# Key transposes moved ahead of the tail's scores in slot 0, with another order of loads, weight splits and the last stores, in a fused attention and two-layer gated network

## The chip, the cores and the metric

One core of a Trainium2 chip runs the whole program. The metric is the device time of one execution in microseconds (us). The engines that matter are TensorE (PE in the rows), VectorE (DVE), ScalarE (ACT), GpSimd (POOL) and SyncE (SP), which issues nearly all DMAs; ACT issues a few weight loads. A matmul streams one operand through weights loaded before and writes PSUM. Each engine runs its own instruction list in order, and semaphores tie the lists together.

## The reference

```python
def _attn_ref(q, k, v):                      # (8, 8, 576, 64) each
    k_p = k.reshape(B, H, Sp, pool, D).mean(axis=3)     # pool 8: 72 keys
    v_p = v.reshape(B, H, Sp, pool, D).mean(axis=3)
    scores = scale * np.matmul(q, k_p.transpose(0, 1, 3, 2))
    scores = scores - np.max(scores, axis=-1, keepdims=True)
    attn = np.exp(scores)
    attn = attn / (np.sum(attn, axis=-1, keepdims=True) + 1e-09)
    return np.matmul(attn, v_p)
...
x = attn_out.transpose(0, 2, 1, 3).reshape(B * S, H * D)    # 4608 x 512
h = x @ w_in1                                # 512 -> 2048
g = where(h >= 1, h, where(h <= -1, 0, (h + 1) ** 2 / 4))
x = g @ w_out1                               # 2048 -> 512
h = x @ w_in2;  g = h / (1 + exp(-h));  out = g @ w_out2
```

## The kernel before

All products of the two layers are made in three passes over operands split into a high and a low part: `hi*hi`, `hi*lo`, `lo*hi` (`three_passes`, L676 to L678). ScalarE makes the high part (`split_high`, `split_input`, `gate_high`), VectorE or GpSimd subtracts it from the raw value for the low part (`split_low`, `gate_low`).

The 4608 tokens form nine blocks of 512; there are 18 block passes, nine for layer 1 and nine for layer 2. A block pass has 16 steps `s`. In each, PE makes hidden chunk `s` (12 matmuls into `ps_h`) and the output product of chunk `s-2` (12 matmuls into the four banks of `ps_y`), while DVE, ACT and POOL turn `ps_h` into the gate's high and low parts. The layers hand over through `y_dram`, the attention hands over through `x_dram`.

The attention of batch `b` is spread over the layer 1 pass of block `b`. Its work is cut into pieces, and the table `PIECES` gives each piece a slot; there are two slots for each step. Each batch has five units `u`: unit 0 is the tail of 64 tokens of this batch, units 1 to 4 are pairs of heads of the next batch. "S" is a unit's scores (PE), maximum and subtraction (`take`, DVE), exponential (ACT), and in the slot behind, `normalise` and `turn_probs` (DVE). "V" is its product with the values (PE) and `copy_output` (ACT), "Q" turns the next queries (`turn_queries`, DVE), and "K" transposes the next batch's pooled keys on PE (`turn_keys`, L604) and copies them to `kT` (`copy_keys`, ACT). S of unit `u` sits in slot `5u`, V in `5u+7`; K sits in slot 2. All share the two PSUM banks `ps_a`; scores use columns 0 to 287 of each, and the keys have been turned into columns 0 to 287 of bank 1, which is why `turn_keys` waits until the tail's scores are taken out. Probabilities go out to `p_dram` and come back transposed as `pT` (`put_probs`, `take_probs`), since the DMA does part of the turning.

Block 0 has an order of its own (`first_block`, `first_gates`, the `FIRST_*` tables): weights are still being loaded and split, and four attention units are made before it. In it, PE walks the slots through `first_slot`, and ACT and DVE follow in `first_gates` and then in `one_block(..., start=6)`. `FIRST_LOW_DVE` says after which step DVE splits which weight piece.

SP's list sets the order of the DMAs: `first_attention_dmas` and `attention_dmas` for the two kinds of block, then `store_y`. SP waits in place, so a DMA behind a waiting one is issued later. The second layer's weights are loaded during block 8 through a ring of three places (`load_weight`), 24 pieces (`SWAP_TAIL`) in that block; then SP loads the first input of layer 2 (`load_x(blocks, y_dram, 0, half)`). A block's result leaves `ps_y` through two buffers of `y_sb`, ACT's and DVE's in turn (`copy_y`, L924 and L1154); each second copy waits until the store out of its buffer has landed.

Of the kernel before, what the change touches and what calls it, by code (L numbers as in the profile page):

```python
# [8 lines left out]
ACT = mybir.ActivationFunctionType  # L9
AXIS_X = mybir.AxisListType.X  # L10

P = 128
BLOCK = 512
POOL = 8
PAIRS = 4
# [13 lines left out]
UNITS = 5  # L29
PIECES = {2: [("K", 0), ("Q", 0)]}  # L30
# [36 lines left out]
FIRST_LOW_DVE = {4: (10,), 5: (14, 16), 7: (19,), 8: (21,), 9: (23,), 10: (25,), 11: (27,), 12: (29,),  # L67
# [12 lines left out]
def build(nc, q, k, v, w_in1, w_out1, w_in2, w_out2, x_dram, y_dram, out):  # L80
# [12 lines left out]
    with ExitStack() as ctx:  # L93
# [73 lines left out]
        early_o = [ps_h[:, 0, :], ps_h[:, 1, :], ps_h[:, 0, :], ps_y[:, 0, :]]  # L167

# [70 lines left out]
        def unit(b, u):  # L239

            return 5 * b + (PAIRS + 1 + u)
# [120 lines left out]
        def _(sp):  # L362
# [115 lines left out]
            def first_attention_dmas():  # L478
# [18 lines left out]
                put_probs(0, 3)  # L497
                sp.wait_ge(kv_added, 12)
                load_kv(k, 2, 0)
                store_pair(0, 1, 1)  # L500
                take_probs(0, 3)
# [11 lines left out]
                sp.wait_ge(kv_added, 18)  # L513
                load_kv(v, 2, 0)
# [47 lines left out]
            store_y(0, 0, 0)  # L562
            with sp.Fori(1, batches - 1) as b:
                attention_dmas(b, (b + 2) % batches)
                store_y(b, b, 0)
# [7 lines left out]
            for i in range(SWAP_TAIL):  # L573
                load_weight(sp, W_PIECES + i)
            for half in range(2):
                load_x(blocks, y_dram, 0, half)
            store_y(blocks - 1, blocks - 1, 0)
# [13 lines left out]
            store_y(2 * blocks - 1, blocks - 1, 1)  # L591
# [8 lines left out]
        def _(pe):  # L600
# [232 lines left out]
        def _(act):  # L833
# [20 lines left out]
            def copy_keys(b, u):  # L854
                act.wait_ge(kT_made, b + (PAIRS + 1))
                for r in range(2):
                    rows = slice(r * dim, (r + 1) * dim)
                    turned = ps_a[rows, 1, 0:PAIRS * keys].rearrange("p (c k) -> p c k", k=keys)
                    nc.scalar.activation(kT[rows, :, r, :], turned, ACT.Copy).then_inc(kT_copied, 1)
# [25 lines left out]
            task_of = {"K": copy_keys, "S": exponential, "V": copy_output}  # L885

            def attention_slot(b, slot, most):
                for kind, u in PIECES.get(slot, ()):
                    if kind in task_of and u < most and not (kind == "K" and most == 1):
                        task_of[kind](b, u)  # L890

# [41 lines left out]
            def first_gates():  # L933
# [11 lines left out]
                attention_slot(0, 2, UNITS)  # L945
# [8 lines left out]
            def one_block(B, layer, units=0, loads=lambda s: (), more=True, start=0):  # L954
                for s in range(start, FC):
                    before, behind = slots_of(B, s)
                    gate_begin(B, s, layer)
                    for slot in before:
                        attention_slot(B, slot, units)
# [11 lines left out]
                copy_y(B)  # L971
# [68 lines left out]
        def _(dve):  # L1040
# [104 lines left out]
            def copy_y(B, units):  # L1145
                if units > 0:
                    dve.wait_ge(x_stored, 80 * B + 16 * units)
                for i in range(2):
                    if i == 0:
                        dve.wait_ge(y_done, B * 3 + 2)  # L1150
                    else:
                        dve.wait_ge(l2_done, B * FC + FC)
                    dve.wait_ge(y_stored[1], B * 32 + 16 * (i + 1))
                    nc.vector.tensor_copy(y_sb[:, 1, :], ps_y[:, 2 * i + 1, :]  # L1154
                                          ).then_inc(y_copied_dve, 1)
# [23 lines left out]
            def one_block(B, layer, units=0, loads=lambda s: (), more=True, start=0):  # L1179
# [15 lines left out]
                copy_y(B, units)  # L1195
# [140 lines left out]
```

## Time and profile before

| what | value |
|---|---|
| three runs | 1694.07, 1694.46, 1699.36 us; median 1694.46 |
| the profiled execution | 1694.82 us, its span 1693.0 us |
| PE busy | 1673.6 us, 99% of the span |
| DVE, ACT, POOL busy | 685.2, 507.5, 545.3 us |
| TensorE's granted clock, mean | 0.998 |
| from the tail's scores of block 2 to those of block 3 | 98.54 us |

The span runs from the first to the last instruction; the remaining 1.8 us of the execution lie outside it. PE being busy at 99% says that only its few idle stretches, its time at a lower clock, and the time before its first and behind its last matmul can be shortened without taking matmuls away.

### The profile page before, as it was taken

How to read it: one execution, taken by the hardware profiler on the slowest of the kernel's cores; microseconds unless marked ns; L12 is line 12 of the kernel's file. 1: busy time of each engine (PE TensorE's matmuls, PEld its weight loads, DVE VectorE, ACT ScalarE, POOL GpSimd, SP SyncE). 2: the span in 40 equal slices, each digit the busy share in tenths (PEclk: the TensorE clock that was granted, in tenths of full speed). 3: DMA queues.
4: the chain of work that ended last, by engine and by line, in shares of the span. 5: the costliest groups of instructions: out<-in, count | busy, mean ns of one | idle time of the engine just before them, and what ended most of it. 6: DMA issues, size and time to landing. Idle time of an engine off the chain costs nothing.

```text
span 1693.0 us, 21063 instructions
## 1 busy us (share of the span) xinstructions
PE 1673.6 (99%) x7588; PEld 1355.9 (80%) x7588; DVE 685.2 (40%) x900; ACT 507.5 (30%) x856; POOL 545.3 (32%) x418
## 2 busy tenths in 40 slices
PE   8999999999999999999999999999999999999998
PEld 6777777787877778788887888888888888888887
DVE  7866656475765647442464221212121212121211
ACT  5442232332323233232344222322232223222222
POOL 6653524244352434322222222222222222222221
PEclk9999999999999999999999999999999999999999
DMA  8654525344352534420123110101010101010000
GB/s 217 165 152 97 127 69 121 95 100 110 82 129 65 121 96 100 110 62 1 59 97 112 32 50 1 50 0 50 0 50 0 50 0 50 0 50 0 25 0 25
DMA packets 139799, 114.99 MB, mean 68 GB/s; under 512 B 86676, under 2 KB 95892, under 8 KB 139764
## 3 DMA queue, kind: packets, MB, share of 16 engines
q1 hardware_dynamic: 138036, 111.38, 24.6%
q10 hardware_dynamic: 1728, 3.15, 0.6%
q8 instruction: 21, 0.34, 0.1%
q14 instruction: 14, 0.11, 0.0%
HBM read 74.65 MB, written 39.85 MB: 68 GB/s over the span
## 4 chain that ended last, share of the span: by engine, by line
PE 93%; DVE 2%; DMA 2%; SPq 1%; issue 0%; ACT 0%; POOL 0%; DVEq 0%; ACTq 0%
PE ps_h L676 15%; PE ps_y L676 15%; PE ps_h L677 15%; PE ps_h L678 15%; PE ps_y L678 15%; PE ps_y L677 15%; PE ps_a L646 2%; PE ps_a L617 2%; DMA second_k<-in_k_dram 1%; PE ps_a L633 0%; DMA pT<-p_dram 0%; DVE win_lo L1047 0%; SPq L397 0%; SPq L378 0%; DMA x_raw<-y_dram 0%
## 5 line engine op out<-in xcount | busy, mean ns | idle before, releaser
L1269 POOL TENSOR_TENSOR g_lo<-g_tmp,g_hi 128x512 fp32r<-128x512 f32 x286 | 369.9, 1293 | 1100.2 <-ACT g_hi L915 1100.2
L676 PE MATMUL ps_h<-x_hi,win_hi 128*128 128x512 f32 x1144 | 451.5, 395 | 0.5 <-DVE g_tmp L1139 0.3
L677 PE MATMUL ps_h<-x_lo,win_hi 128*128 128x512 f32 x1144 | 446.2, 390 | 0.0
L678 PE MATMUL ps_h<-x_hi,win_lo 128*128 128x512 f32 x1144 | 445.9, 390 | 0.0
L1143 DVE TENSOR_TENSOR g_tmp<-g_tmp,ps_h 128x512 f32<-128x512 f32 x144 | 99.0, 688 | 577.4 <-ACT g_tmp L905 577.4
L676 PEld LDWEIGHTS ps_h<-x_hi,win_hi 128*128 128x128 f32 x1144 | 215.2, 188 | 58.1 <-issue 12.2
L678 PEld LDWEIGHTS ps_h<-x_hi,win_lo 128*128 128x128 f32 x1144 | 215.2, 188 | 45.4
L677 PEld LDWEIGHTS ps_h<-x_lo,win_hi 128*128 128x128 f32 x1144 | 215.1, 188 | 43.0
L915 ACT ACTIVATE g_hi<-g_tmp 128x512 fp32r<-128x512 f32 x286 | 180.5, 631 | 225.7 <-DVE g_tmp L1139 121.4
L676 PE MATMUL ps_y<-g_hi,wout_hi 128*128 128x512 f32 x576 | 227.8, 395 | 1.0 <-POOL g_lo L1269 1.0
L678 PE MATMUL ps_y<-g_hi,wout_lo 128*128 128x512 f32 x576 | 224.3, 389 | 0.0
L677 PE MATMUL ps_y<-g_lo,wout_hi 128*128 128x512 f32 x576 | 224.3, 389 | 0.0
L676 PE MATMUL ps_y<-wout_hi,g_hi 128*128 128x512 f32 x576 | 224.1, 389 | 0.0
L677 PE MATMUL ps_y<-wout_lo,g_hi 128*128 128x512 f32 x576 | 224.1, 389 | 0.0
L678 PE MATMUL ps_y<-wout_hi,g_lo 128*128 128x512 f32 x576 | 224.1, 389 | 0.0
L905 ACT ACTIVATE g_tmp<-ps_h 128x512 f32<-128x512 f32 x144 | 86.1, 598 | 420.5 <-PE ps_h L678 420.5
L908 ACT ACTIVATE g_tmp<-g_tmp 128x512 f32<-128x512 f32 x142 | 89.7, 632 | 363.3 <-DVE g_tmp L1132 363.3
L1132 DVE TENSOR_SCALAR g_tmp<-ps_h 128x512 f32<-128x512 f32 x142 | 96.9, 683 | 207.8 <-PE ps_h L678 207.5
L676 PEld LDWEIGHTS ps_y<-g_hi,wout_hi 128*128 128x128 f32 x576 | 108.1, 188 | 35.8 <-issue 13.0
L678 PEld LDWEIGHTS ps_y<-g_hi,wout_lo 128*128 128x128 f32 x576 | 108.1, 188 | 23.1
L677 PEld LDWEIGHTS ps_y<-wout_lo,g_hi 128*128 128x128 f32 x576 | 108.3, 188 | 22.5
L676 PEld LDWEIGHTS ps_y<-wout_hi,g_hi 128*128 128x128 f32 x576 | 108.1, 188 | 22.4
(121 smaller groups left out, 1246.1 us busy)
## 6 DMA issues: line engine op xcount, KB each, us to landing
p_dram<-x_raw SPq DMA_DIRECT2D x28, 384.0 KB, 2.3
y_dram<-y_sb SPq DMA_DIRECT2D x36, 256.0 KB, 2.1
x_raw<-y_dram SPq DMA_DIRECT2D x18, 512.0 KB, 4.2
out_dram<-y_sb SPq DMA_DIRECT2D x36, 256.0 KB, 2.1
kv_raw<-in_k_dram SPq DMA_DIRECT2D x15, 576.0 KB
kv_raw<-in_v_dram SPq DMA_DIRECT2D x15, 576.0 KB
x_raw<-x_dram SPq DMA_DIRECT2D x16, 512.0 KB, 4.1
q_pair<-in_q_dram SPq DMA_DIRECT2D x120, 64.0 KB, 4.8
```

The costliest lines, as they stand in the source:

```text
L617: last = mm(banks[:, t // 2, at:at + 2 * keys], qT[:, t * P:(t + 1) * P], kT[:, c, :, :].rearrange("p r k -> p (r k)"), start=True, stop=True)
L646: last = mm(bank[r * dim:(r + 1) * dim, :], v_sum[:, 2 * c + r, :], probs[:, r], start=True, stop=True)
L676: mm(dst, w_h, a_h, start=first, stop=False)
L677: mm(dst, w_h, a_l, start=False, stop=False)
L678: return mm(dst, w_l, a_h, start=False, stop=last)
L905: nc.scalar.activation(t, ps_h[:, s % 2, :], ACT.Sigmoid).then_inc(sigmoid_done, 1)
L908: nc.scalar.activation(t, t, ACT.Square, bias=1.0).then_inc(square_done, 1)
L915: nc.scalar.activation(g_hi[:, s % G_BUFS, :], t, ACT.Copy).then_inc(g_hi_done, 1)
L1132: nc.vector.tensor_scalar(t, bank_of(B, s), -1.0, 1.0, ALU.max, ALU.min).then_inc(ramp_done, 1)
L1143: nc.vector.tensor_tensor(t, t, h, ALU.mult).then_inc(g_done, 1)
L1269: nc.gpsimd.tensor_tensor(g_lo[:, s % G_BUFS, :], gate_place(B, s), g_hi[:, s % G_BUFS, :].bitcast(F32), ALU.subtract).then_inc(g_lo_done, 1)
```

## The change

The order is changed in six places.

1. `PIECES`: K goes from slot 2 to slot 0, ahead of the tail's scores. The keys are turned into columns 288 to 431 of both `ps_a` banks, two head pairs in each, so PE no longer waits there for the scores to be taken. ACT copies them in slot 1.
2. In block 0, SP issues the store of pair 1 and the three loads of `pT` for unit 3 ahead of a load of pooled keys' input that waits for POOL.
3. Behind block 0, SP issues the four `y` stores ahead of the load of values that waits for POOL's last sum.
4. In block 0, DVE splits weight piece 16 one step later, and ACT runs the slots in front of a step's gate ahead of `gate_begin` (not behind it).
5. In block 8, SP loads the first input of layer 2 ahead of the last six of the 24 weight pieces.
6. The last block's result is copied into the four chunks of `x_raw`, not the two buffers of `y_sb`, so that no copy waits for a store.

```diff
-PIECES = {2: [("K", 0), ("Q", 0)]}
+PIECES = {0: [("K", 0)], 2: [("Q", 0)]}
...
-FIRST_LOW_DVE = {4: (10,), 5: (14, 16), 7: (19,), 8: (21,), 9: (23,), 10: (25,), 11: (27,), 12: (29,),
+FIRST_LOW_DVE = {4: (10,), 5: (14,), 6: (16,), 7: (19,), 8: (21,), 9: (23,), 10: (25,), 11: (27,), 12: (29,),
...
+        turned_keys = ps_a[:, :, 4 * keys:6 * keys].rearrange("p g (c k) -> p g c k", k=keys)
...
                 put_probs(0, 3)
+                store_pair(0, 1, 1)
+                take_probs(0, 3)
                 sp.wait_ge(kv_added, 12)
                 load_kv(k, 2, 0)
-                store_pair(0, 1, 1)
-                take_probs(0, 3)
...
-                sp.wait_ge(kv_added, 18)
-                load_kv(v, 2, 0)
+
+            def store_last_y():
+                for d in range(4):
+                    sp.wait_ge((y_copied_act, y_copied_dve)[d % 2], 2 * (2 * blocks - 1) + d // 2 + 1)
+                    at = (blocks - 1) * BLOCK + d * P
+                    sp.dma_start(out[at:at + P, :], x_raw[:, d, :]).then_inc(y_stored[d % 2], 16)
...
             store_y(0, 0, 0)
+            sp.wait_ge(kv_added, 18)
+            load_kv(v, 2, 0)
...
-            for i in range(SWAP_TAIL):
+            for i in range(SWAP_TAIL - 6):
                 load_weight(sp, W_PIECES + i)
             for half in range(2):
                 load_x(blocks, y_dram, 0, half)
+            for i in range(SWAP_TAIL - 6, SWAP_TAIL):
+                load_weight(sp, W_PIECES + i)
...
             def turn_keys(b, u):
                 pe.wait_ge(kv_added, 12 * b + 6)
-                pe.wait_ge(scores_taken, unit(b, 0))
+                pe.wait_ge(o_copied, 5 * b)
                 for c in range(PAIRS):
-                    last = transpose_keys(ps_a[:, 1, c * keys:(c + 1) * keys], c)
+                    last = transpose_keys(turned_keys[:, c // 2, c % 2, :], c)
...
             def copy_keys(b, u):
                 act.wait_ge(kT_made, b + (PAIRS + 1))
+                act.wait_ge(scores_taken, unit(b, 0))
...
+                if ("K", 0) in PIECES.get(slot - 1, ()) and most > 1:
+                    copy_keys(b, 0)
...
-            def copy_y(B):
+            def copy_y(B, more):
...
-                    act.wait_ge(y_stored[0], B * 32 + 16 * (i + 1))
-                    nc.scalar.activation(y_sb[:, 0, :], ps_y[:, 2 * i, :], ACT.Copy
-                                         ).then_inc(y_copied_act, 1)
+                    if more:
+                        act.wait_ge(y_stored[0], B * 32 + 16 * (i + 1))
+                    elif i == 0:
+                        act.wait_ge(x_lo_done, 2 * blocks * KC)
+                    dst = y_sb[:, 0, :] if more else x_raw[:, 2 * i, :]
+                    nc.scalar.activation(dst, ps_y[:, 2 * i, :], ACT.Copy).then_inc(y_copied_act, 1)
...
                     before, behind = slots_of(B, s)
+                    if start:
+                        for slot in before:
+                            attention_slot(B, slot, units)
                     gate_begin(B, s, layer)
-                    for slot in before:
-                        attention_slot(B, slot, units)
+                    if not start:
+                        for slot in before:
+                            attention_slot(B, slot, units)
```

VectorE's `copy_y` is changed as ScalarE's is.

Order on PE at the start of a pass of the batch loop, before. L633 is the tail's scores, L604 the key transposes, and the two are one hidden chunk apart:

```order
L622 ISA
L633 MATMUL ps_a<-kT,qT 64x144 x4
L676 MATMUL ps_h<-x_hi,win_hi 128x512
L677 MATMUL ps_h<-x_lo,win_hi 128x512
...
L608 ISA
L609 REGISTER_ALU
L604 MATMUL ps_a<-ident,k_sum 128x72 x4
L691 ISA
L676 MATMUL ps_h<-x_hi,win_hi 128x512
```

The same place now (L615 are the transposes, L644 the scores):

```order
L619 ISA
L620 REGISTER_ALU
L615 MATMUL ps_a<-ident,k_sum 128x72 x4
L633 REGISTER_ALU
L644 MATMUL ps_a<-kT,qT 64x144 x4
L687 MATMUL ps_h<-x_hi,win_hi 128x512
```

The transposes have moved one hidden chunk forward, in front of the scores, and no wait for the scores stands between chunks 1 and 2 any more.

Order on SP at the end of block 0 before. The names are the DRAM and SBUF tensors; the `kv_raw` rows are loads of keys or values, the `y_sb` row the block's four stores:

```order
L371 DMA kv_raw<-in_k_dram 72x4x512
L420 DMA x_dram<-y_sb 128x512
L437 DMA x_raw<-x_dram 128x2x512
L371 DMA kv_raw<-in_v_dram 72x4x512
L524 DMA y_dram<-y_sb 128x512 x4
```

And now:

```order
L374 DMA kv_raw<-in_k_dram 72x4x512
L423 DMA x_dram<-y_sb 128x512
L440 DMA x_raw<-x_dram 128x2x512
L531 DMA y_dram<-y_sb 128x512 x4
L374 DMA kv_raw<-in_v_dram 72x4x512
```

The load of values, with its wait for POOL, has gone behind the stores. Order on DVE in steps 5 and 6 of block 0, before (L1047 are weight splits, L1132 begins a gate, L1090 turns queries):

```order
L1058 TENSOR_TENSOR prob<-ps_a,row_max 128x8x72
L1047 TENSOR_TENSOR win_lo<-w_early,win_hi 128x512
L1047 TENSOR_TENSOR win_lo<-w_raw,win_hi 128x512
L1063 TENSOR_REDUCE row_sum<-prob 128x8
...
L1132 TENSOR_SCALAR g_tmp<-ps_h 128x512
L1090 STREAM_TRANSPOSE qT<-q_pair 128x512
```

And now:

```order
L1072 TENSOR_TENSOR win_lo<-w_early,win_hi 128x512
L1088 TENSOR_REDUCE row_sum<-prob 128x8
...
L1157 TENSOR_SCALAR g_tmp<-ps_h 128x512
L1115 STREAM_TRANSPOSE qT<-q_pair 128x512
...
L1083 TENSOR_TENSOR prob<-ps_a,row_max 128x8x72
L1072 TENSOR_TENSOR win_lo<-w_raw,win_hi 128x512
```

The second split (piece 16) has moved behind the next unit's subtraction.

## Rows read from the trace of the kernel before

**Rows 1.** Page, part 1: busy time, share, instructions of each engine.
```profile
PE 1673.6 (99%) x7588; PEld 1355.9 (80%) x7588; DVE 685.2 (40%) x900; ACT 507.5 (30%) x856; POOL 545.3 (32%) x418
```
**Rows 2.** Waits of PE: us in total, times, longest (four of the 14 rows).
```profile
PE ps_a L604 <- DVE prob L1058: 2.2, 1, 2.2
PE ps_a L617 <- ACT y_sb L878: 2.0, 1, 2.0
...
PE ps_a L646 <- DMA pT<-p_dram: 1.1, 1, 1.1
PE ps_y L676 <- POOL g_lo L1269: 1.0, 1, 1.0
```
**Rows 3.** Chain of work, the tail's scores in blocks 1, 2, 3: start, us, what.
```profile
133.68 1.12 PE ps_a L633 x8
...
236.53 1.12 PE ps_a L633 x8
...
335.07 1.12 PE ps_a L633 x8
```
**Rows 4.** Windows: length, busy (x) by engine, PEclk, DMA share, GB/s.
```profile
140.00:145.00 5.00, 4.88 (x17) 3.82 (x18) 4.71 (x7) 1.12 (x2) 1.27 (x1) 0.66 0.00 0
```
**Rows 5.** Timeline, 130 to 140 us (block 1 begins): start, us, what, [idle before <-releaser].
```profile
130.14 0.32 SPq L371 DMA_DIRECT2D kv_raw<-in_v_dram  x1
...
130.50 7.68 SPq L524 DMA_DIRECT2D y_dram<-y_sb  x4
...
137.13 0.69 DVE L1154 COPY y_sb<-ps_y 128x512 f32<-128x512 f32 x1 [6.75 <-DMA y_dram<-y_sb]
...
137.74 0.68 DVE L1132 TENSOR_SCALAR g_tmp<-ps_h 128x512 f32<-128x512 f32 x1
...
139.92 0.47 PE L604 MATMUL ps_a<-ident,k_sum 72*128 72x72 f32 x4 [2.17 <-DVE prob L1058]
```
**Rows 6.** Timeline, 232 to 241 us, the same place in block 2.
```profile
232.57 4.14 SPq L524 DMA_DIRECT2D y_dram<-y_sb  x4
...
239.15 0.67 DVE L1139 SCALAR_TENSOR_TENSOR g_tmp<-g_tmp,ps_h 128x512 f32<-128x512 f32 x1
...
240.44 0.41 PE L604 MATMUL ps_a<-ident,k_sum 72*128 72x72 f32 x4
...
240.66 0.48 PE L676 MATMUL ps_h<-x_hi,win_hi 128*128 128x512 f32 x1
...
240.98 0.40 PE L677 MATMUL ps_h<-x_lo,win_hi 128*128 128x512 f32 x1
```
**Rows 7.** Timeline, 57 to 84 us, block 0 from step 5 on.
```profile
57.88 4.27 DVE L1047 TENSOR_TENSOR win_lo<-w_raw,win_hi 128x512 fp32r<-128x512 f32 x1
...
60.31 1.28 POOL L1269 TENSOR_TENSOR g_lo<-g_tmp,g_hi 128x512 fp32r<-128x512 f32 x1
...
65.29 0.65 DVE L1132 TENSOR_SCALAR g_tmp<-ps_h 128x512 f32<-128x512 f32 x1
...
83.02 0.70 DVE L1047 TENSOR_TENSOR wout_lo<-w_early,wout_hi 128x512 fp32r<-128x512 f32 x1
```
**Rows 8.** Timeline of SP, 94 to 97 us (block 0).
```profile
94.44 0.31 SPq L371 DMA_DIRECT2D kv_raw<-in_k_dram  x1
...
95.23 1.91 SPq L414 DMA_DIRECT2D pT<-p_dram  x3
```
**Rows 9.** Windows of 100 us: around the change of layer, and inside layer 2.
```profile
814.00:914.00 100.00, 98.92 (x435) 81.08 (x434) 51.41 (x66) 40.79 (x69) 23.23 (x18) 1.00 0.31 102
1078.00:1178.00 100.00, 100.00 (x442) 82.83 (x442) 18.84 (x27) 27.13 (x45) 24.51 (x19) 1.00 0.12 42
```
**Rows 10.** Timeline around 898 us and at the end.
```profile
898.18 1.16 ACT L896 ACTIVATE x_hi<-x_raw 128x512 fp32r<-128x512 f32 x2 [1.96 <-DMA x_raw<-y_dram]
...
1687.80 0.39 PE L678 MATMUL ps_y<-wout_hi,g_lo 128*128 128x512 f32 x1
...
1689.75 0.69 DVE L1154 COPY y_sb<-ps_y 128x512 f32<-128x512 f32 x1 [2.20 <-DMA out_dram<-y_sb]
```

More of the change, by code:

```diff
@@ L590, in _ @@
                 block_dmas(b)
-            store_y(2 * blocks - 1, blocks - 1, 1)
+            store_last_y()
             sp.wait_ge(kv_landed, 16 * (4 * batches - 2))
@@ L855, in copy_keys @@
                 act.wait_ge(kT_made, b + (PAIRS + 1))
+                act.wait_ge(scores_taken, unit(b, 0))
                 for r in range(2):
                     rows = slice(r * dim, (r + 1) * dim)
-                    turned = ps_a[rows, 1, 0:PAIRS * keys].rearrange("p (c k) -> p c k", k=keys)
-                    nc.scalar.activation(kT[rows, :, r, :], turned, ACT.Copy).then_inc(kT_copied, 1)
+                    nc.scalar.activation(kT[rows, :, r, :].rearrange("p (g c) k -> p g c k", g=2),
+                                         turned_keys[rows], ACT.Copy).then_inc(kT_copied, 1)
             def exp_rows(held):
@@ L883, in copy_output @@
                 nc.scalar.activation(dst, src, ACT.Copy).then_inc(o_copied, 1)
-            task_of = {"K": copy_keys, "S": exponential, "V": copy_output}
+            task_of = {"S": exponential, "V": copy_output}
             def attention_slot(b, slot, most):
                 for kind, u in PIECES.get(slot, ()):
-                    if kind in task_of and u < most and not (kind == "K" and most == 1):
+                    if kind in task_of and u < most:
                         task_of[kind](b, u)
+                if ("K", 0) in PIECES.get(slot - 1, ()) and most > 1:
+                    copy_keys(b, 0)
             def split_input(B, half):
@@ L944, in first_gates @@
                 gate_begin(0, 4, 0)
-                attention_slot(0, 2, UNITS)
+                attention_slot(0, 1, UNITS)
                 gate_high(0, 3)
@@ L970, in one_block @@
                         split_high(n)
-                copy_y(B)
+                copy_y(B, more)
             def first_keys(c):
@@ L1143, in gate_end, with copy_y @@
                     nc.vector.tensor_tensor(t, t, h, ALU.mult).then_inc(g_done, 1)
-            def copy_y(B, units):
+            def copy_y(B, units, more):
                 if units > 0:
@@ L1152, in copy_y @@
                         dve.wait_ge(l2_done, B * FC + FC)
-                    dve.wait_ge(y_stored[1], B * 32 + 16 * (i + 1))
-                    nc.vector.tensor_copy(y_sb[:, 1, :], ps_y[:, 2 * i + 1, :]
-                                          ).then_inc(y_copied_dve, 1)
+                    if more:
+                        dve.wait_ge(y_stored[1], B * 32 + 16 * (i + 1))
+                    dst = y_sb[:, 1, :] if more else x_raw[:, 2 * i + 1, :]
+                    nc.vector.tensor_copy(dst, ps_y[:, 2 * i + 1, :]).then_inc(y_copied_dve, 1)
             def first_gates():
@@ L1194, in one_block @@
                     split_input(B + 1)
-                copy_y(B, units)
+                copy_y(B, units, more)
             nc.vector.memset(kT[:], 0.0).then_inc(kT_zero, 1)
```

## Prediction

> **What bounds the kernel now.** The page's busy times come first: PE is busy 1673.6 of 1693.0 us [rows 1], no matmul is taken away, so the change can win only PE's idle time, time at a lower clock, and the tail behind its last matmul. The list of PE's waits, read next, says where the idle time is: four single waits of 2.2, 2.0, 1.1 and 1.0 us, each happening once in the program [rows 2]. None falls in the batch loop from its second pass on. The chain of waits then gives the price of the first one. The tail's scores stand at the same place in each pass, so their distance is the length of a pass: 335.07 - 236.53 = 98.54 us from block 2 to 3, but 236.53 - 133.68 = 102.85 us from block 1 to 2 [rows 3]. Block 1 costs 4.31 us more than its like, though its wait is only 2.2 us. The rest is the clock: between 140 and 145 us the granted clock is 0.66 of full, a mean over stretches at 2.4 GHz and at 1.2 GHz, and 17 matmuls run where 5.00 / 0.2262 = 22 would fit (0.2262 us is 100 us / 442) [rows 4, 9]. It fell right after the 2.17 us of idle.
>
> **The change part by part**, against the profiled execution of 1694.82 us (span 1693.0 and 1.8 around it).
>
> Boundary of blocks 0 and 1 (parts 1 and 3 of the change). PE waits at the key transposes for VectorE's subtraction of the tail's scores. VectorE is late because its gate starts at 137.74, behind the second copy of `y` at 137.13, which sat idle 6.75 us for a store out of its buffer. That store was issued behind a load of values, which SP had held back to 130.14 for POOL's last sum; the four stores took SP 7.68 us from first to last [rows 5]. In block 2, where no such load is ahead, SP needs 4.14 us, and no wait arises [rows 6]. With the stores first, block 1 becomes like block 2. Moving the transposes would remove the named wait alone, but not the late gate, on which hidden chunk 2 waits as well; the two edits have one answer. I take the whole 4.3 us. The bounds: 0 if the stores stay late, 4.31 at most. What is hidden: the values' load now starts some 3 us later, when the last copy is out, and POOL needs it two steps into block 1, which at 98.54 / 16 = 6.2 us a step is over 10 us on; without that cover its lateness would reach PE through POOL's list.
>
> Step 6 of block 0 (part 4). PE waits 2.0 us for ACT's copy of the tail's output [rows 2]. ACT made it behind its gate step, which waited for VectorE's gate begin at 65.29; in front of that VectorE spent 4.27 us on the split of piece 16 [rows 7]. Now the copy goes ahead of the gate step and the split behind the next unit. PE also needs the queries turned by VectorE right behind the gate begin, so the order of ACT alone would give back only part; the split's 4.27 us are the larger term, and 65.29 - 4.27 = 61.0 brings the gate begin forward by more than the wait. I take 2.0. Lower bound 0 (below).
>
> Unit 3's probabilities in block 0 (part 2). PE waits 1.1 us for `pT` [rows 2]. Its loads are issued at 95.23, behind the load of keys' input at 94.44, which itself waited for POOL [rows 8]. Ahead of it, they wait only for the copy of unit 2's output, and do not share the DMA engines with that load. I take the 1.1 and 0.1 for the slower first matmul after a stop: 1.2, between 0 and 1.2. The keys' load slips by about what the store and three loads take to issue, 0.4 + 1.9 us, into POOL's slack.
>
> Change of layer (part 5). ScalarE gets `x_raw` at 898.18 after waiting 1.96 us for a load [rows 10]; the gate's high part of chunk 15 is queued behind it, POOL waits for that, and PE for POOL, 1.0 us [rows 2]. Both following gates are late too. 100 us around this place hold 435 matmuls, 100 us of layer 2 hold 442 [rows 9]: 7 x 0.2262 = 1.6 us. With six weight pieces fewer in front, the load is issued about three steps of 24 matmuls, some 16 us, earlier. I take 1.6 (0 to 1.6). The last six pieces have these 16 us less only by the load's own time; each has a step of slack, so nothing is charged.
>
> The end (part 6). The last matmul starts at 1687.80 and takes 0.39; the last copy starts at 1689.75, having waited 2.20 us for a store [rows 10]. With a place of its own it starts at about 1688.25, and everything behind it is as before: 1.5 us. If four stores so close disturb each other, less: 0.5 as the lower bound.
>
> The loop (part 1). In each of seven blocks the transposes, 240.44 to 240.66, join the scores. The first matmul after them is followed by the next after 0.32 us and not 0.2262 [rows 6]; one such change of kind falls away: 0.09 x 7 = 0.65. Between transposes and scores a new one may arise, so 0 to 1.3, or a loss up to 0.65. The transposes' 0.22 us now stand in front of the scores, and the tail's take, and with it the end of gate 0, come 0.22 to 0.31 us later: 239.15 + 0.67 becomes about 240.1, while chunk 2, which waits for it, starts at about 240.6. The slack of 0.84 shrinks to about 0.5 and holds. ACT's key copies move into a stretch in which it waits for the next gate.
>
> Sum: 4.3 + 2.0 + 1.2 + 1.6 + 1.5 + 0.65 = 11.25 us; 1694.82 - 11.25 = 1683.6 for the profiled execution. The median of the runs is 0.36 below that execution, so 1683.2 us.
>
> The split of piece 16 took 4.27 us while POOL worked without a pause (its row at 60.31 is one of four), and a split of the same size at 83.02 took 0.70 [rows 7]. By the Trainium skill, SBUF — State Buffer, section "SBUF: two separate sides", a VectorE operation with two SBUF inputs and a GpSimd operation that reads SBUF exclude each other for a whole instruction; the trace agrees. By that rule the split can be as long at its new place, since POOL has splits of its own there; the sum would lose up to all of part 4.
>
> **The rivals.**
> A. The split is as long at its new place and delays gate 7 and unit 2's probabilities by 2 to 4.3 us; or the earlier pace of block 0 meets a load that comes no earlier. For it: 4.27 us in a row that has 0.70 elsewhere. Against: the new place has no PE wait near it, and gate 7 is not needed for two steps. Loses 2 to 4.3: 1685.2 to 1687.5, say 1686.2.
> B. The boundary stall stays: the stores land late for another reason, or the gate starts late all the same. For it: four stores are waited for one by one. Against: block 2 does the same in 4.14 us. 1683.2 + 4.3 = 1687.5.
> C. The change of layer gives nothing: the load of 1 MB in front of piece 18 starves ScalarE's next weight split. Against: the ring has a step of slack. 1683.2 + 1.6 = 1684.8, or 1686 with a stall of its own.
> D. Slower: gate 0 falls behind chunk 2 in the batch loop. The slack of 0.84 us is used up by the transposes in front of the scores (a register wait and a new change of kind between them), PE stops by x in each of six passes, and each stop brings the clock down as in block 1, where 4.31 - 2.17 = 2.1 us came on top of the idle time. It costs 6 (x + 2.1) and decides from x = 0.7, where it is 16.8 and outweighs 11.25 by 5.1. With x = 1.0: 1683.8 + 18.6 = 1702.4. Against: 0.31 is the most I find, and it needs over 1.5.
>
> **How the numbers follow.** Forecast 0.72, A 0.13, B 0.05, C 0.04, D 0.06. A measurement of this kernel tells 0.3%, 5.1 us, from no change. The forecast, A, B and C are all more than 5.1 below 1694.5: faster 0.94. D is split between small x (within 0.3%) and larger: same 0.03, slower 0.03. The range takes the forecast with its terms' bounds (1681.5 if the loop gives 1.3 and block 0 another 1 us), A and B: 1681.5 to 1688.0.
>
> **What would show it.** Block 1 as long as block 2, and a granted clock of 1.00 from 140 to 145 us; `y_dram` stores of block 0 over in about 4 us; the PE waits on `pT`, on the tail's copy, on `g_lo` at the change of layer and on VectorE's subtraction gone from the list; 441 or 442 matmuls in the 100 us around the change of layer; the last copy starting 0.1 us behind the last matmul, and the span ending some 3.3 us behind it; block 2 to 3 at about 98.4 us. Wrong: block 2 to 3 above 98.54 (the loop pays), a new PE wait of over 1 us in block 0 (A), or a stretch below full clock.

## The result and the profile after

| | before | after |
|---|---|---|
| runs | 1694.46, 1699.36, 1694.07, 1696.63 us | 1684.07, 1685.51, 1683.99, 1685.45 us |
| median | 1695.55 us | 1684.76 us |
| profiled execution, its span | 1694.82, 1693.0 us | 1684.07, 1682.3 us |

The ratio is 0.9933, with a 95% interval of 0.9914 to 0.9951, so the kernel is faster by more than 0.3%. The profiled executions are 10.75 us apart where the sum gave 11.25. As before [rows 1], the page's part 1 shows no matmul gone. PE is busy 3.1 us less with as many:

```profile
PE 1670.5 (99%) x7588; PEld 1355.7 (81%) x7588; DVE 691.9 (41%) x900; ACT 508.0 (30%) x856; POOL 546.0 (32%) x418
```

The list of PE's waits (us in total, times, longest) answers to [rows 2]. None of the four rows there has a counterpart. The first two rows below are in the opening, and their like was in the list before. The one on `L687` is new and lies behind the change of layer:

```profile
PE ps_a L651 <- DVE prob L1097: 2.8, 1, 2.8
PE ps_h L808 <- POOL ident L1318: 1.5, 1, 1.5
...
PE ps_h L687 <- DVE g_tmp L1168: 0.2, 1, 0.2
```

The chain of work gives the length of a pass as in [rows 3]. From the tail's scores of block 1 to those of block 2 it is now 98.53 us, not 102.85, and from block 2 to 3 98.54, as before:

```profile
130.22 1.12 PE ps_a L644 x8
...
228.75 1.12 PE ps_a L644 x8
...
327.29 1.12 PE ps_a L644 x8
```

The windows of [rows 4] and [rows 9], the columns being busy time (count) of PE, weight loads, DVE, ACT and POOL, then granted clock, DMA share and GB/s. The clock at the boundary is 1.00 where it was 0.66, and 441 matmuls, not 435, run around the change of layer:

```profile
140.00:145.00 5.00, 5.00 (x26) 4.25 (x25) 4.01 (x7) 3.03 (x5) 3.76 (x3) 1.00 0.28 56
814.00:914.00 100.00, 99.80 (x441) 82.32 (x440) 53.59 (x67) 42.44 (x72) 25.49 (x20) 1.00 0.28 94
```

The timeline around 130 us answers to [rows 5]. The four stores are issued first and take SP 5.64 us (about 4 were forecast), and DVE's second copy has waited 3.79 us, not 6.75. The gate's first operation starts behind that copy at 131.06, which is 0.84 us after the scores' place in the chain (130.22). It was 4.06 before (137.74 against 133.68). The load of values comes last:

```profile
125.86 5.64 SPq L531 DMA_DIRECT2D y_dram<-y_sb  x4
...
130.15 1.19 PE L644 MATMUL ps_a<-kT,qT 128*64 128x144 f32 x8
...
130.45 0.69 DVE L1181 COPY y_sb<-ps_y 128x512 f32<-128x512 f32 x1 [3.79 <-DMA y_dram<-y_sb]
...
131.06 0.68 DVE L1157 TENSOR_SCALAR g_tmp<-ps_h 128x512 f32<-128x512 f32 x1
...
131.54 0.40 SPq L374 DMA_DIRECT2D kv_raw<-in_v_dram  x1
```

The end answers to [rows 10]. The last copy starts 0.42 us behind the start of the last matmul, where it was 1.95:

```profile
1678.53 0.39 PE L689 MATMUL ps_y<-wout_hi,g_lo 128*128 128x512 f32 x1
...
1678.95 0.69 DVE L1181 COPY x_raw<-ps_y 128x512 f32<-128x512 f32 x1 [0.67 <-PE ps_y L689]
```

Where the 10.75 us came from is seen by the length of each block pass, counted from the start of its first hidden matmul to that of the next pass (18 passes of 384 matmuls of 512 columns each):

| stretch, us | before | after | gained | forecast |
|---|---|---|---|---|
| up to the first hidden matmul | 24.22 | 24.19 | 0.03 | 0 |
| block 0 | 106.58 | 102.89 | 3.69 | 3.2 + 0.1 |
| block 1 | 102.85 | 98.54 | 4.31 | 4.3 |
| blocks 2 to 6, sum | 492.70 | 492.81 | -0.11 | 0.5 |
| block 7 | 89.43 | 89.43 | 0.00 | 0 |
| blocks 8 and 9, sum | 175.92 | 174.57 | 1.35 | 1.6 |
| last matmul's start to the span's end | 5.23 | 3.75 | 1.48 | 1.5 |

Blocks 10 to 17 have the same lengths before and after.

### The profile page after: what moved, and what is told of

It reads as the page before. It is cut to its first block, busy times and chain, and to the rows that moved or that the text cites. A ratio compares the mean times of both kernels' runs of the same rounds, so it can differ in the third digit from the quotient of the medians.

```text
span 1682.3 us, 21073 instructions
## 1 busy us (share of the span) xinstructions
PE 1670.5 (99%) x7588; PEld 1355.7 (81%) x7588; DVE 691.9 (41%) x900; ACT 508.0 (30%) x856; POOL 546.0 (32%) x418
## 4 chain that ended last, share of the span: by engine, by line
PE 98%; DVE 1%; DMA 0%; ACT 0%; issue 0%; DVEq 0%; ACTq 0%
PE ps_y L687 16%; PE ps_h L687 16%; PE ps_y L689 16%; PE ps_y L688 16%; PE ps_h L688 15%; PE ps_h L689 15%; PE ps_a L657 2%; PE ps_a L628 2%; PE ps_a L644 1%; PE ps_a L674 0%; DMA y_dram<-y_sb 0%; DMA early_k<-in_k_dram 0%; PE ps_a L651 0%; PE ps_y L628 0%; PE ps_h L657 0%
## 5 line engine op out<-in xcount | busy, mean ns | idle before, releaser
L687 PE MATMUL ps_h<-x_hi,win_hi 128*128 128x512 f32 x1144 | 450.2, 394 | 0.2 <-DVE g_tmp L1168 0.2
L687 PEld LDWEIGHTS ps_h<-x_hi,win_hi 128*128 128x128 f32 x1144 | 214.7, 188 | 57.4 <-issue 12.1
L687 PE MATMUL ps_y<-g_hi,wout_hi 128*128 128x512 f32 x576 | 227.6, 395 | 0.0
L687 PE MATMUL ps_y<-wout_hi,g_hi 128*128 128x512 f32 x576 | 224.1, 389 | 0.0
L687 PEld LDWEIGHTS ps_y<-g_hi,wout_hi 128*128 128x128 f32 x576 | 108.1, 188 | 34.6 <-issue 13.0
L687 PEld LDWEIGHTS ps_y<-wout_hi,g_hi 128*128 128x128 f32 x576 | 108.2, 188 | 22.5
```

The source lines that it names most:

```text
L687: mm(dst, w_h, a_h, start=first, stop=False)
```

## The experiments

Below, a kernel named "alone" is the kernel before with one part of the change. Block lengths are counted as in the table above. The first three kernels below were timed six times each on one chip, beside 11 runs of before (median 1693.65 us). Their ratios to it are 0.9956 (the changed kernel), 0.9951 and 0.9949, each with an interval about 0.0028 wide. The kernels with one part alone ran once each, so their total times are not compared here, only the passes in their traces. Four of them (the split, ACT's order, unit 3's probabilities and the stores) ran on a chip where the one run of before took 1699.10 us, which was not traced.

### The changed kernel again

No edit.

> The changed kernel itself, timed beside the next ones. Its first four runs lie in two groups, 1684.0 with a mean clock of 1.000 and 1685.5 with 0.999. If this is a property of the kernel, both groups come again, 1.4 to 1.5 us apart; if it was the chip or the hour, one group.

Median 1687.09 us of six runs from 1685.65 to 1688.30, ratio 0.9956 (0.9942 to 0.9969). They form neither two groups nor one as narrow as that of the four runs above. The profiled execution took 1688.30 us and had its first hidden matmul at 28.19 us, not 24.19: PE spent part of the opening at half clock, as the window's clock of 0.75 shows.

```profile
10.00:35.00 25.00, 20.09 (x100) 14.47 (x99) 17.56 (x29) 13.69 (x26) 17.09 (x21) 0.75 0.98 263
```

From there on its blocks are as those of the first profile, but for block 6, 98.93 with a wait for `pT`, and block 9, 87.93. So of the 4.2 us between the two profiled executions 4.0 lie in the opening, which no part of the change touches.

### All but part 1 (keys in slot 2)

```diff
-PIECES = {0: [("K", 0)], 2: [("Q", 0)]}
+PIECES = {2: [("K", 0), ("Q", 0)]}
...
-                    last = transpose_keys(turned_keys[:, c // 2, c % 2, :], c)
+                    last = transpose_keys(ps_a[:, 1, c * keys:(c + 1) * keys], c)
...
```

ACT's key copies and the wait of the transposes are put back with it.

> Everything of the change but part 1: the key transposes stay in slot 2 in the old columns and wait for the tail's scores to be taken. Theory: the boundary was mended by the order of the stores alone. Block 1 then lasts 98.5 us as now, and the time is that of the changed kernel within 0.5 us: it loses 0.06 us a block by the two separate groups on PE, and wins back the new waits for pT at unit 1 (0.06 to 0.24 us in blocks 2, 5 and 6), which come from the tail's scores standing 0.35 us later. Rival: the move of the transposes carries the 4.3 us; then block 1 is 100 to 103 us again and the time 1686 to 1688.

Median 1686.31 us (1684.56 to 1688.42), ratio 0.9951 (0.9938 to 0.9965): not to be told from the changed kernel on the same chip. From the scores of block 1 to those of block 2 it is 98.86 us:

```profile
133.04 1.19 PE L644 MATMUL ps_a<-kT,qT 128*64 128x144 f32 x8
...
231.90 1.19 PE L644 MATMUL ps_a<-kT,qT 128*64 128x144 f32 x8
```

The boundary is mended to within 0.3 us by the order of stores. Blocks 2 to 5 take 98.54 each, 0.07 more than with part 1. Block 6 takes 99.09, with a wait that part 1 therefore does not cause. It is that of unit 1's product with the values (the tile's row on the timeline, releaser in brackets):

```profile
658.27 1.08 PE L657 MATMUL ps_a<-pT,v_sum 72*64 72x512 f32 x4 [0.44 <-DMA pT<-p_dram]
```

### Unit 1's probabilities ahead of the values' load

The changed kernel with, in each pass of the batch loop:

```diff
                 put_probs(b, 1)
-                sp.wait_ge(kv_added, 12 * b + 9)
-                load_kv(v, n, 1)
                 store_tail(b)
                 take_probs(b, 1)
+                sp.wait_ge(kv_added, 12 * b + 9)
+                load_kv(v, n, 1)
```

> The changed kernel, and in the batch loop SP issues the tail's store and the loads of pT for unit 1 ahead of the load of values that waits for POOL (it stood in front of them). Theory: the new PE waits before unit 1's product are waits for pT to land; they go, blocks 2, 5 and 6 fall to 98.47 like 3 and 4, 0.3 to 0.5 us less in all, and if the slower group of runs comes from such waits growing, that group goes too. Rival: they are something else on PE's queue (the profile names no releaser); then they stay.

Median 1685.19 us (1682.86 to 1687.59), ratio 0.9949 (0.9934 to 0.9963). No wait for `pT` is left, and blocks 1 to 6 all take 98.47 us:

```profile
130.03 1.12 PE ps_a L644 x8
...
228.50 1.12 PE ps_a L644 x8
...
326.96 1.12 PE ps_a L644 x8
```

In the changed kernel the load of values was issued ahead of these. In its first profile block 5 is 0.24 us longer than the shortest pass. PE stood idle there for 0.14 us ahead of the product, which came 8.3 us behind the start of the issue of the three `pT` loads. The trace names no releaser for this wait; it names the `pT` load for the longer ones in block 6 of two other executions (0.39 us in the changed kernel again, 0.44 above):

```profile
546.35 0.32 SPq L374 DMA_DIRECT2D kv_raw<-in_v_dram  x1
546.87 0.42 SPq L431 DMA_DIRECT2D x_dram<-y_sb  x1
547.40 1.36 SPq L417 DMA_DIRECT2D pT<-p_dram  x3
...
555.74 1.08 PE L657 MATMUL ps_a<-pT,v_sum 72*64 72x512 f32 x4
```

### Part 1 alone

```diff
-PIECES = {2: [("K", 0), ("Q", 0)]}
+PIECES = {0: [("K", 0)], 2: [("Q", 0)]}
...
```

The other edits of part 1, to the transposes and to ACT's key copies, are in it too.

> The kernel before with part 1 alone: transposes in slot 0, in the free columns. Theory: the wait at the transposes goes from the list, but the late gate still stops PE at hidden chunk 2, at about the same time. Block 1 stays near 102.8 us, with the clock down again; the time is within 0.7 us of before. Rival: moving the transposes mends the boundary by itself; block 1 falls to 98.5 and the time by 4.3 us.

One run, 1697.31 us. The named wait of the transposes is gone, and another of 2.76 us stands in its place: hidden chunk 2, waiting for the gate that starts late. The scores of blocks 1 and 2 are 103.15 us apart:

```profile
135.88 1.19 PE L635 MATMUL ps_a<-kT,qT 128*64 128x144 f32 x8
...
142.78 0.50 PE L678 MATMUL ps_h<-x_hi,win_hi 128*128 128x512 f32 x1 [2.76 <-DVE g_tmp L1144]
...
239.03 1.19 PE L635 MATMUL ps_a<-kT,qT 128*64 128x144 f32 x8
```

Blocks 2 to 5 take 98.47, as they should by part 1, and block 6 takes 99.21, with a wait of 0.66 us for `pT`. Block 0 is longer too, 108.82 us. PE's wait at unit 2's scores was 2.71 us there, and behind it the granted clock was 0.60 and then 0.55 in the stretches from 68 to 72 us. The split of piece 16 was long here too, and its rows are read further below:

```profile
58.57 1.73 POOL L329 TENSOR_TENSOR kv_raw<-kv_raw 72x512 f32<-72x512 f32 x1
59.07 4.25 DVE L1052 TENSOR_TENSOR win_lo<-w_raw,win_hi 128x512 fp32r<-128x512 f32 x1
60.26 1.28 POOL L1274 TENSOR_TENSOR g_lo<-g_tmp,g_hi 128x512 fp32r<-128x512 f32 x1
61.50 1.27 POOL L1265 TENSOR_TENSOR win_lo<-w_raw,win_hi 128x512 fp32r<-128x512 f32 x1
```

### The split of piece 16 alone

```diff
-FIRST_LOW_DVE = {4: (10,), 5: (14, 16), 7: (19,), ...
+FIRST_LOW_DVE = {4: (10,), 5: (14,), 6: (16,), 7: (19,), ...
```

> The kernel before with the first half of part 4 alone: VectorE splits weight piece 16 one step later. Theory: with the 4.27 us split out of the way the gate begin and the turned queries of step 6 come 3 to 4 us earlier, and ScalarE's copy with them, so PE's wait at unit 2's scores (2.0 us) goes: block 0 falls from 106.6 to about 104.6 us. By the rule that VectorE and GpSimd exclude each other, the split may last over 3 us at its new place too, where no PE wait follows. Rival: ScalarE's order is what counts; then the wait stays at over 1 us.

One run, 1691.53 us. The wait of unit 2's scores is gone and block 0 takes 103.71 us. Much of the step from 106.58 is not the edit's, since before itself takes 104.19 in a second execution (below), and 0.5 us under that is what the edit can claim. At its new place the split took 1.40 us:

```profile
66.95 1.40 DVE L1047 TENSOR_TENSOR win_lo<-w_raw,win_hi 128x512 fp32r<-128x512 f32 x1
```

### ACT's order alone (the rest of part 4)

```diff
+                    if start:
+                        for slot in before:
+                            attention_slot(B, slot, units)
                     gate_begin(B, s, layer)
-                    for slot in before:
-                        attention_slot(B, slot, units)
+                    if not start:
+                        for slot in before:
+                            attention_slot(B, slot, units)
```

> The kernel before with the second half of part 4 alone: in block 0 from step 6 ScalarE copies the unit's output ahead of its gate step. Theory: PE also needs the queries that VectorE turns behind its gate begin at 65.3 us, so only the last 0.5 us of the 2.0 us wait go: block 0 106.0 to 106.2 us. Rival: the copy alone was missing; block 0 falls by 2.0 us to 104.6.

One run, 1691.32 us, and the wait of unit 2's scores is gone here too, with block 0 at 104.25. But in this execution the split of piece 16, still at its old place, took 1.77 us and not 4.27. In the executions where it is as short, the wait is 0.3 us. ACT's order removes it, but block 0 gets no shorter (104.19 to 104.24 in three executions that have it), because PE then waits longer for `pT`, 1.24 us where those have 0.65 to 0.75:

```profile
101.42 1.08 PE L646 MATMUL ps_a<-pT,v_sum 72*64 72x512 f32 x4 [1.24 <-DMA pT<-p_dram]
```

What this order would do behind a split of 4.27 the run does not show.

### Unit 3's probabilities alone (part 2)

```diff
                 put_probs(0, 3)
+                store_pair(0, 1, 1)
+                take_probs(0, 3)
                 sp.wait_ge(kv_added, 12)
                 load_kv(k, 2, 0)
-                store_pair(0, 1, 1)
-                take_probs(0, 3)
```

> The kernel before with part 2 alone: the pT loads of unit 3 in block 0 ahead of the load of keys' input. Theory: the wait for pT of 1.1 us goes, block 0 falls from 106.6 to 105.4 us, nothing else moves. Rival: the loads are slow for their own sake and the wait stays in part.

One run, 1693.21 us. The wait for `pT` is gone, and block 0 takes 103.44 us. Three executions that keep that wait (0.65, 0.69 and 0.75 us) and have the same 0.3 us at unit 2's scores take 104.19, 104.24 and 104.20.

### The stores alone (part 3)

```diff
-                sp.wait_ge(kv_added, 18)
-                load_kv(v, 2, 0)
...
             store_y(0, 0, 0)
+            sp.wait_ge(kv_added, 18)
+            load_kv(v, 2, 0)
```

> The kernel before with part 3 alone: the four stores of block 0 ahead of the load of values. Theory: block 1 falls from 102.85 to 98.54 us, no clock fall there, the stores take SP about 4 to 5 us and not 7.7. Rival: the stores were slow for another reason, or the transposes' wait for the tail's scores keeps a stop; then block 1 stays above 100 us.

One run, 1691.90 us. Neither a wait of the transposes nor a lower clock is left at the boundary, and the scores of blocks 1 and 2 are 98.99 us apart. The load of values is issued at 136.46, behind the stores. Both rows of scores, and SP's:

```profile
134.71 1.19 PE L633 MATMUL ps_a<-kT,qT 128*64 128x144 f32 x8
...
233.70 1.19 PE L633 MATMUL ps_a<-kT,qT 128*64 128x144 f32 x8
```

```profile
130.68 5.74 SPq L522 DMA_DIRECT2D y_dram<-y_sb  x4
...
136.46 0.42 SPq L371 DMA_DIRECT2D kv_raw<-in_v_dram  x1
```

The traces also tell why the stores were late. In the seven executions with the load of values ahead, the first store was issued 0.28 or 0.29 us before block 1 begins and landed 5.7 to 6.3 us later. In the seven with the stores ahead, it was issued 1.22 us before and landed in 2.0 to 4.0. So SP's own wait cost 0.9 us, and the larger part came after the issue, while the load was ahead of the stores in the DMA queue. Which step of the DMA held them there is not shown.

### The kernel before again

No edit.

> The kernel before, a second profile. In three kernels whose block 0 is unchanged at unit 2's scores, PE's wait for ScalarE's copy there was 2.7, 0.3 and 0.3 us where the first profile of before had 2.0. Theory: this wait depends on how VectorE's split of piece 16 falls between GpSimd's instructions, and so differs from run to run; it will be 0.3 to 2.7 us here, and the split's row long or short with it. Rival: 2.0 us again, and the others differ by their edits. Block 1 is 102 to 102.9 us either way.

One run, 1695.23 us. Three sizes differ from the execution on which the forecast rests. The opening took 28.29 us, not 24.22, for PE ran at half rate in part of it. The clock is not on record here before 21.28 us, but eight matmuls of one shape took 2.29 us in it and later 1.22:

```profile
8.59 2.29 PE L617 MATMUL ps_y<-kT,qT 128*128 128x144 f32 x8 [0.69 <-ACT qT L984]
...
26.45 1.22 PE L617 MATMUL ps_y<-kT,qT 128*128 128x144 f32 x8 [0.20 <-DVE prob L1072]
```

The split of piece 16 took 1.77 us, not 4.27, and the wait of unit 2's scores 0.33, not 2.0 (here with the releaser in brackets), so block 0 took 104.19 and not 106.58:

```profile
61.67 1.77 DVE L1047 TENSOR_TENSOR win_lo<-w_raw,win_hi 128x512 fp32r<-128x512 f32 x1
...
69.27 0.97 PE L617 MATMUL ps_a<-kT,qT 128*128 128x144 f32 x6 [0.33 <-ACT y_sb L878]
```

And the boundary's wait of 2.0 us brought no lower clock with it. The window has 1.00, and block 1 took 101.71, not 102.85:

```profile
140.00:145.00 5.00, 3.42 (x17) 2.78 (x18) 4.71 (x7) 1.85 (x3) 1.28 (x1) 1.00 0.18 68
```

### The input of layer 2 alone (part 5)

```diff
-            for i in range(SWAP_TAIL):
+            for i in range(SWAP_TAIL - 6):
                 load_weight(sp, W_PIECES + i)
             for half in range(2):
                 load_x(blocks, y_dram, 0, half)
+            for i in range(SWAP_TAIL - 6, SWAP_TAIL):
+                load_weight(sp, W_PIECES + i)
```

> The kernel before with part 5 alone: the first input of layer 2 loaded ahead of the last six weight pieces. Theory: the wait for POOL at the end of block 8 (1.0 us) goes and block 8 falls from 88.36 to 87.04 us; block 9 keeps up to 0.9 us, since its first gate also waits for the stores of block 8's result. Rival: the pieces behind the input land late and ScalarE's weight splits stop PE in block 8 or 9.

One run, 1690.81 us. Block 8 fell to 87.04 us, the length of an undisturbed layer 2 pass; it was 88.37 in both executions of before. Block 9 took 88.25, where those had 87.55 and 87.38. So the two blocks together gained only 0.5 to 0.6 us here. In block 9's first steps the waits list has a row of 0.9 us for DVE's gate operation:

```profile
PE ps_h L678 <- DVE g_tmp L1145: 0.9, 1, 0.9
```

The timeline shows what held that operation back. ACT's second copy of `y` waited 4.48 us for a store, ACT's table load and gate step came behind the copy, and DVE waited for ACT:

```profile
902.69 0.60 ACT L926 ACTIVATE y_sb<-ps_y 128x512 f32<-128x512 f32 x1 [4.48 <-DMA y_dram<-y_sb]
903.31 1.28 ACT L907 ACT_TABLE_LOAD   x1
904.61 0.60 ACT L907 ACTIVATE g_tmp<-ps_h 128x512 f32<-128x512 f32 x1
...
905.23 0.69 DVE L1145 TENSOR_TENSOR g_tmp<-g_tmp,ps_h 128x512 f32<-128x512 f32 x1 [1.23 <-ACT g_tmp L907]
```

The store in question is ACT's first of this block. It landed 4.4 us after its issue, where it took 2.0 in before. In the six executions that have part 5 and not the edit of the next section it took 3.2 to 4.4 us.

### A version with both remaining waits mended

The changed kernel with unit 1's probabilities ahead of the values' load, as above, and with the last two weight splits that DVE makes in block 8 put between its two copies of `y`, where it would wait for the store anyway. The edit of `copy_y` and of its caller:

```diff
-            def copy_y(B, units, more):
+            def copy_y(B, units, more, between=()):
...
                     nc.vector.tensor_copy(dst, ps_y[:, 2 * i + 1, :]).then_inc(y_copied_dve, 1)
+                    for n in between if i == 0 else ():
+                        split_low(n)
...
-                    for n in loads(s):
+                    late = loads is swap_loads and s == FC - 1
+                    for n in () if late else loads(s):
                         split_low(n)
...
-                copy_y(B, units, more)
+                copy_y(B, units, more, swap_loads(FC - 1) if loads is swap_loads else ())
```

> A version meant to beat both: the changed kernel with (a) SP's tail store and pT loads of unit 1 ahead of the load of values in the batch loop, and (b) in block 8 VectorE's last two weight splits between its two copies of y and not ahead of them, so that the first store leaves 1.3 us earlier. Theory: blocks 2 to 6 are 98.47 us each, block 9 is 87.04 to 87.1 with no wait on VectorE's first gate of layer 2, and the time is 0.8 to 1.3 us below the changed kernel beside it. Rival: the opening of the program differs by more from run to run than both edits give, and the two cannot be told apart.

And the changed kernel beside it:

> The changed kernel on the same chip, for the comparison with the version beside it: its runs spread over 1684 to 1688 us by the start of the first hidden product (24.2 us in one execution, 28.2 in another) and by the clock before it, while blocks 1 to 17 are the same within 0.5 us a block.

The mended version has a median of 1683.82 us of six runs (1683.23 to 1685.81), the changed kernel 1685.59 (1685.23 to 1686.33), and before 1695.49 (11 runs). The ratios to before are 0.9934 (0.9917 to 0.9951) and 0.9944 (0.9928 to 0.9961). Five of the six runs of the mended version are below all six of the changed kernel's. In its profile blocks 1 to 6 take 98.47 us and blocks 8 and 9 87.04 each. The changed kernel, too, has 98.47 in blocks 1 to 6 here, with no wait for `pT`, and 87.36 in block 9. So the edits are worth 0.3 us in the two profiled executions, out of 1.8 between the medians. The opening gave another 0.8 in the two profiled executions (first hidden matmul at 25.57 against 26.39), which is no merit of the edit, as the clocks of the two windows show:

```profile
10.00:35.00 25.00, 19.80 (x105) 13.34 (x106) 19.44 (x30) 14.81 (x28) 20.07 (x23) 0.93 0.99 258
```

```profile
10.00:35.00 25.00, 20.46 (x103) 13.38 (x103) 19.02 (x29) 14.15 (x26) 19.28 (x22) 0.86 1.00 247
```

The rest of the 1.8 us is not shown to come from the edits, and the intervals of the two ratios overlap.

## Why the prediction was right

**The boundary, 4.3 us: right, and by the cause that was named.** Block 1 gained 4.31 us. The stores alone take block 1 to 98.99 and the transposes alone leave it at 103.15 with the wait under another name. So the term belongs to part 3; part 1 adds the last 0.3 to 0.5 (98.86 and 98.99 without it, 98.54 with it). Of that the list of waits names 0.16 us in one of the two, unit 1's scores waiting for ACT's copy of the turned keys, and no owner of the rest. But 4.3 is the price in an execution where the clock falls. In four executions whose boundary wait of 2.0 to 2.5 us left the clock at 1.00, block 1 took 101.6 to 102.2, so the same edit is worth 3.1 to 3.7 us in those. That corrects one reading of the prediction, which put all of the 2.1 us beyond the idle time down to the clock. In each of these four, 1.1 to 1.2 us beyond the wait are lost at a clock of 1.00 (before again: 101.71 - 98.54 - 2.03 = 1.14), so about 1 us of the 2.1 was the clock's.

**Step 6 of block 0, 2.0 us: right for the two executions compared, and partly luck.** The waits of 2.0 and 2.7 us come with a split of 4.27 and 4.25 us; in five other executions with the split at its old place it took 1.77 and the wait was 0.3 or, with ACT's new order, none. The term is worth 0.3 to 0.5 us or over 2, and the profile used was one of the two of seven with the long split. Whether the split's place or ACT's order does it when the split is long was not separated. With the short split, the new place alone brings block 0 from 104.19 to 103.71, and ACT's order alone brings nothing (104.25).

**Unit 3's probabilities, 1.2 us: the wait is gone, in the changed kernel and with part 2 alone.** Together with step 6 the forecast was 3.2, with 0.1 of the loop term 3.3, and block 0 gained 3.69. Of the 0.4 more, 0.25 is a wait at 40.97 us for DVE's gate, which only the two executions with the long split have and which no part of the change was meant for. By itself part 2 gave 0.75 us (104.19 to 103.44), against a wait of 0.7 in that comparison; the wait was 1.1 in the profile used. Against 104.19 the whole change gains 1.3 us in block 0, not 3.69.

**The change of layer, 1.6 us: 1.35.** The mechanism holds for block 8, which takes 87.04 us in all seven executions with part 5 and 88.37 to 88.93 in the seven without. What the count of matmuls hid is that the two passes had different owners. Without part 5 block 9 takes 87.04 to 87.55 us, and in the longest of these DVE's gate operation comes directly behind its second `y` copy. With part 5 it takes 87.11 to 88.25 (87.53 here), and the owner is ACT's second copy, held up by a store that lands 3.2 to 4.4 us after its issue. So part 5 can give back a part of its gain one block later. With the two splits moved, DVE's first store is issued 0.8 us behind ACT's and not 2.1, ACT's lands in 2.05 us, and block 9 takes 87.04, in one execution. Why that store was slow is not shown.

**The end, 1.5 us: 1.48.** The lower bound for stores that disturb each other was not needed. No kernel has part 6 alone, but from the last matmul's start to the span's end it is 3.74 to 3.75 us in the six executions with it and 5.22 to 5.23 in the eight without.

**The loop, 0.65 us: the step that failed.** I took one change of kind as falling away in each pass, 0.09 us, and named a new one between transposes and scores only as a bound. It does arise. Before, the scores started 0.32 us behind the matmul of 512 columns ahead of them, and the first such matmul behind the transposes was followed by the next after 0.32. Now the scores start 0.35 us behind the first of the transposes:

```profile
228.11 0.39 PE L689 MATMUL ps_h<-x_hi,win_lo 128*128 128x512 f32 x1
228.34 0.41 PE L615 MATMUL ps_a<-ident,k_sum 72*128 72x72 f32 x4
228.69 1.19 PE L644 MATMUL ps_a<-kT,qT 128*64 128x144 f32 x8
229.81 0.50 PE L687 MATMUL ps_h<-x_hi,win_hi 128*128 128x512 f32 x1
```

Matmul by matmul the four transposes start 61 to 65 ns apart, and the first of the scores 157 ns behind the last of them. A pass gains 0.07 us: 98.54 to 98.47. Over seven passes that is 0.5 us and not 0.65, which is the part of the miss that belongs to the step. Of it nothing is left in blocks 2 to 6 in sum in the first profile, because three of the five are 0.06, 0.24 and 0.16 us longer than 98.47, at unit 1's product with the values. Such delays come and go from execution to execution. In the changed kernel beside the version above there is none, and blocks 2 to 6 take 492.33 us, 0.37 less than before. They are there without part 1 as well: 0.44 us in all but part 1, and in the kernel before with the split's place alone 0.72. With three loads moved in SP's list both executions have none, but one of three of the changed kernel has none either, so that the move removes them is likely and not shown.

**The rivals.** A did not come: the split took 1.81 us at its new place and no wait of PE lies near it. B did not: block 1 is as long as block 2. C did not as stated (block 8 gained its 1.33 us in full), though half a microsecond is lost in block 9. D did not: no pass of the loop is longer than 98.71 us in the first profile, and no wait of PE for gate 0 is in the loop of any profile. D's price was also added up wrongly (6 x 2.8 = 16.8 outweighs 11.25 by 5.55, not 5.1) and rested on 2.1 us for a fall of the clock, of which about 1 is the clock's. Two of the signs named beforehand did not come either: the stores took SP 5.64 us and not about 4, and from block 2 to 3 it is 98.54 us and not 98.4.

**The median.** 1684.76 against 1683.2, within the range. The sum was missed by 0.5: the loop gave 0.6 less and the change of layer 0.25 less, and block 0 gave 0.4 more, which hid some of it. The rest is what a single profiled execution cannot tell: executions of one kernel begin their hidden matmuls anywhere from 24.2 to 28.3 us, before as after. On the two other chips the changed kernel's medians were 1685.59 and 1687.09. There the medians of before and after are 9.9 and 6.6 us apart, and here 10.8. So that 11.25 fits this well is in part luck: the profile it was read from had both the long split and the fall of the clock, and before again had neither.

## What to carry to other kernels

Price a stall that happens once by comparing the pass it lies in with an undisturbed pass, and look for what makes the releaser late: moving the waiting instruction only gives the wait another name. A load that waits for a slow producer does not belong ahead of stores or small loads that others wait for, in a queue that is issued in order; the two edits of that kind gave nearly half of the 10.75 us between the two profiles. And before a term is taken from one execution, ask whether its row is as long elsewhere, since 1.77 or 4.27 us for the same instruction decided whether step 6 was worth 0.3 us or 2.

## What the runs showed of the hardware

- **DVE's split and POOL.** In the rows of part 1 alone above, three POOL operations follow one another from 58.57 to 62.77, and the split, begun at 59.07, ends at 63.32, 0.55 us behind the last of them. It missed the changes from one POOL operation to the next at 60.3 and 61.5. In the kernel before run again it ends at 63.44, 0.55 us behind a POOL operation's end at 62.89, and the POOL operation begun there took 1.74 us, against 1.28 for its like. A split of the same size alone takes 0.70 [rows 7]. The Trainium skill, SBUF — State Buffer, section "SBUF: two separate sides", has whichever starts second fully blocked, of a VectorE operation with two SBUF inputs and a GpSimd operation that reads SBUF, while the first runs its whole instruction. The trace agrees that it is blocked, but it does not always get in when the first is done: in two executions it missed two openings, in five it took the first that came, as this one does:

```profile
61.15 1.74 POOL L1260 TENSOR_TENSOR wout_lo<-w_early,wout_hi 128x512 fp32r<-128x512 f32 x1
61.67 1.77 DVE L1047 TENSOR_TENSOR win_lo<-w_raw,win_hi 128x512 fp32r<-128x512 f32 x1
62.85 1.74 POOL L327 TENSOR_TENSOR kv_raw<-kv_raw 72x512 f32<-72x512 f32 x1
```

- **The clock.** A stop of PE of 2.0 to 2.8 us at the block boundary was followed by a lower granted clock in three executions (stops of 2.17, 2.39 and 2.76 us) and by none in four (1.96, 2.03, 2.30 and 2.52 us). So the length of the stop alone does not decide it. The pass was 4.2 to 4.7 us longer with the lower clock, and 3.1 to 3.7 us without. In block 0 the stop of 2.71 us in part 1 alone brought the clock down, and the one of 2.0 us in the kernel before did not.
- **Stores.** The last four stores of 128 x 512 fp32, issued within 2.47 us, each land 2.0 to 2.2 us after their issue, as they do when spread over 3.7 us in the kernel before (2.0 to 2.1). The same store took 5.7 to 6.3 us to land at the boundary with a load of values issued ahead of it.
